# Attention, then a routed expert layer, then a dense layer on one core: two expert tiles filled from six batches run beside the last routing, and expert 0's weights are split inside the attention loop

## The reference, cut to what matters

```
scores = scale * x @ state.T ; a = softmax(scores) ; xread = a @ state
scores2 = scale * state @ x.T ; a2 = softmax(scores2) ; sread = a2 @ x
x = rows of concatenate([xread, sread]) : 4352 x 512

logits = normalise(x) @ normalise(expert_emb).T / tau
expert_idx = argmax(logits) ; gate_w = softmax(logits)[expert_idx]
for e in range(8):
    h = maximum(x[mask_e] @ w1[e], 0)
    out[mask_e] = gate_w * (h @ w2[e])

h = x @ w_in ; r = maximum(h, 0) ; out = (s * r * r + b) @ w_out
```

## Time and profile before

| | |
|---|---|
| median of 3 runs | 1479.9 us (1479.68 to 1480.39) |
| the profiled execution | 1480.5 us |
| its span, first to last instruction | 1478.8 us |
| granted TensorE clock, mean | 0.965 of full speed |
| tiles of the expert stage | 38 |

### The profile page before, as it was taken

How to read it: one execution, slowest core, us unless ns; L and a number is a source line. 1 busy time by engine, 2 the same in 40 slices (tenths; PEclk the granted TensorE clock), 3 DMA queues, 4 the chain that set the end, 5 groups by cost and what they waited for, 6 DMA issues and landing times.

```text
span 1478.8 us, 22719 instructions
## 1 busy us (share of the span) xinstructions
PE 1365.8 (92%) x6878; PEld 1118.7 (76%) x6879; DVE 651.3 (44%) x1646; ACT 509.1 (34%) x977; POOL 149.0 (10%) x196
## 2 busy tenths in 40 slices
PE   5887459999999999997999999999999999999995
PEld 4655338877787877876888888888888888888884
DVE  4776653566664466465632422423223232322322
ACT  3544413455453355353422222222222222222221
POOL 1222310000000000004000100101001010100101
PEclk9988669999999999999999999999999999999998
DMA  9745333144433144214010010101001010010000
GB/s 218 147 112 79 65 106 120 51 150 172 172 115 101 44 161 146 80 52 153 24 44 0 24 34 0 57 0 57 0 0 57 0 57 0 21 36 0 29 1 28
DMA packets 75154, 100.19 MB, mean 68 GB/s; under 512 B 43977, under 2 KB 44521, under 8 KB 74097
## 3 DMA queue, kind: packets, MB, share of 16 engines
q1 hardware_dynamic: 62448, 69.72, 16.7%
q0 software_dynamic: 7200, 20.08, 4.1%
q10 hardware_dynamic: 5472, 9.96, 1.8%
HBM read 71.24 MB, written 28.66 MB: 68 GB/s over the span
## 4 chain that ended last, share of the span: by engine, by line
PE 74%; DVE 7%; DMA 5%; issue 5%; ACT 3%; DVEq 2%; ACTq 1%; POOL 1%; SPq 0%; another core or an unknown queue 0%; POOLq 0%
PE bank_a L1357 25%; PE bank_n L1376 13%; PE bank_t L1376 12%; PE bank_a L1290 9%; PE bank_n L1316 8%; DMA xg<-x_tok,g_idx 3%; PE bank_t L1301 1%; DMA slot_tab<-ids,pos 1%; DMA x_tok<-st_rows 1%; DVEq L339 1%; PE bank_a L1102 1%; PE bank_n L1276 1%; DVEq L336 1%; PE bank_t L1119 1%; DVE w_lo L970 1%
## 5 line engine op out<-in xcount | busy, mean ns | idle before, releaser
L1054 DVE TENSOR_TENSOR sq<-rel 128x512 f32<-128x512 f32 (+1 forms) x144 | 95.5, 663 | 484.8 <-ACT rel L714 484.8
L714 ACT ACTIVATE rel<-bank_a 128x512 f32<-128x512 f32 (+1 forms) x144 | 82.8, 575 | 549.6 <-PE bank_a L1357 549.6
L1357 PE MATMUL bank_a<-y_hi,w_in_hi 128*128 128x512 f32 (+1 forms) x576 | 218.6, 379 | 7.1 <-DVE y_lo L1046 7.0
L1357 PE MATMUL bank_a<-y_hi,w_in_lo 128*128 128x512 f32 (+1 forms) x576 | 217.9, 378 | 0.0
L1357 PE MATMUL bank_a<-y_lo,w_in_hi 128*128 128x512 f32 (+1 forms) x576 | 217.8, 378 | 0.0
L1357 PEld LDWEIGHTS bank_a<-y_hi,w_in_hi 128*128 128x128 f32 x576 | 109.0, 189 | 28.7 <-DVE y_lo L1046 7.5
L1357 PEld LDWEIGHTS bank_a<-y_lo,w_in_hi 128*128 128x128 f32 x576 | 109.0, 189 | 20.7 <-issue 0.2
L1357 PEld LDWEIGHTS bank_a<-y_hi,w_in_lo 128*128 128x128 f32 x576 | 108.9, 189 | 19.9
L1316 PE MATMUL bank_n<-w_hi,hid_hi 128*128 128x512 f32 x304 | 118.4, 389 | 1.9 <-DVE hid_lo L977 1.9
L1316 PE MATMUL bank_n<-w_hi,hid_lo 128*128 128x512 f32 x304 | 118.3, 389 | 0.0
L1376 PE MATMUL bank_n<-wo_hi,g_hi 128*128 128x512 f32 x288 | 112.6, 391 | 0.2 <-DVE g_lo L1057 0.2
(11 more groups left out here) (202 smaller groups left out, 2065.7 us busy)
## 6 DMA issues: line engine op xcount, KB each, us to landing
w_raw<-in_moe_w SPq DMA_DIRECT2D x16, 2048.0 KB, 9.3
moe_tok<-yg ACTq DMA_DIRECT2D x38, 256.0 KB, 2.0
x_tok<-x_rows SPq DMA_DIRECT2D x8, 1088.0 KB
x_m<-in_x SPq DMA_DIRECT2D x8, 1024.0 KB
y_rows<-moe_tok SPq DMA_DIRECT2D x8, 1024.0 KB
win_raw<-in_moe_w_in SPq DMA_DIRECT2D x8, 512.0 KB, 8.9
w_raw<-in_moe_w_out SPq DMA_DIRECT2D x1, 4096.0 KB
slot_tab<-ids,pos POOLq DMA_INDIRECT x40
```

The source lines that it names most:

```text
L714: nc.scalar.activation(rel[:, k, 0:cols], ps_g[k][:, 0:cols], ACT.Relu).then_inc(rel_ready, 1)
L1054: nc.vector.tensor_tensor(sq[:, 0:cols], rel[:, k, 0:cols], rel[:, k, 0:cols], ALU.mult).then_inc(sq_ready, 1)
L1357: last = nc.tensor.matmul(ps_g[n % 2][:, 0:cols], w[:, wc], a[:, c, 0:cols], start=(c == 0 and w is w_in_hi and a is y_hi), stop=(c == DC ...
```

## The change

The changed kernel does four things.

1. **Two early tiles.** Tiles 0 and 1 are filled with the first 256 slots of expert 0 as they stand after batches 0 to 5. SP reads these 256 words (`idx_soon`) after it has stored batch 6, POOL gathers tiles 0 and 1 before it writes the slots of batch 7, and PE, ACT and DVE do these tiles between the steps of the last routing. A correction (`room`, `late`, `first_e`) keeps the table right where expert 0 has fewer than 256 tokens so far; with these inputs `room` is 0 and there are 38 tiles as before. `place` has three more small steps at batch 6 and one more at batches 6 and 7.
2. **Expert 0's weights.** `split_hi(i)` and `split_lo(i)` stand in iteration i of the attention loop, one quarter of w1 or w2 in each, on ACT behind the exponential of `e1` and on DVE behind the quotient of `e1`.
3. **The order of a tile.** DVE does `gate_scale(g+2)` straight after `x_lo(g+2)`, where it did `gate_scale(g+3)` behind `hidden_lo(g+1)`; `gate_final` comes last. The split of `w_in` moves from `next_w1` to `next_w2` on ACT and DVE, and SP loads w2 ahead of `w_in`. SP loads `w_out` after the first `y_rows` and not before them.
4. **Setting up.** POOL writes the constants `first_e` and `late` with four small memsets, and DVE waits for them (`tab_zero`, 8) ahead of the loop.

The diff, cut to its core:

```diff
@@ gpsimd @@
             pool.wait_ge(tab_zero, 4)
             pool.wait_ge(tab_cleared, 16)
-            for bb in range(B):
+            nc.gpsimd.memset(first_e[:], 0.0).then_inc(tab_zero, 1)
+            pool.wait_ge(tab_zero, 5)
+            nc.gpsimd.memset(first_e[:, 0:1], 1.0).then_inc(tab_zero, 1)
+            nc.gpsimd.memset(late[:], 1.0).then_inc(tab_zero, 1)
+            pool.wait_ge(tab_zero, 7)
+            nc.gpsimd.memset(late[:, 0:EARLY], 0.0).then_inc(tab_zero, 1)
+
+            def write_slots(bb):
                 pool.wait_ge(pos_ready, bb + 1)
...
+            for bb in range(B - 1):
+                write_slots(bb)
+            pool.wait_ge(soon_loaded, 16)
+            pool.wait_ge(rows_stored, 16 * SOON)
+            pool.wait_ge(st_stored, 16 * SOON)
+            gather(0)
+            gather(1)
+            write_slots(B - 1)
             pool.wait_ge(rows_stored, 16 * B)
             pool.wait_ge(st_stored, 16 * B)
+            pool.wait_ge(tab_ready, 1)
             pool.wait_ge(idx_ready, 1)
...
@@ vector @@
             dve.wait_ge(const_ready, CONSTS + 2)
             dve.wait_ge(hot_zero, 4)
+            dve.wait_ge(tab_zero, 8)
             for i in range(B):
...
                 nc.vector.tensor_tensor(e1_r, e1_r, r1[:].unsqueeze(2).to_broadcast([P, TPB * H, NS]), ALU.mult)\
                     .then_inc(a1_norm, 1)
+                split_lo(i)
                 if i >= 1:
                     state_logits(i - 1)
                     choose(i - 1)
...
             place(B - 2)
             token_rows(B - 1)
             state_logits(B - 1)
+            dve.sem_inc(hid_t_ready, HB)
+            gate_logits(0)
+            x_lo(0)
             choose(B - 1)
+            gate_scale(0)
             place(B - 1)
+            gate_logits(1)
+            x_lo(1)
+            hidden_lo(0)
+            gate_final(0)
...
+            gate_scale(1)
+            hidden_lo(1)
+            next_w1(1)
+            gate_logits(2)
+            x_lo(2)
+            gate_final(1)
+            gate_scale(2)
+            gate_logits(3)
+            gate_final(2)
+            x_lo(3)
...
             def tile(g):
                 x_lo(g + 2)
+                gate_scale(g + 2)
                 next_w1(g + 1)
-                gate_final(g + 2)
                 gate_logits(g + 3)
                 hidden_lo(g + 1)
-                gate_scale(g + 3)
                 next_w2(g)
-
-            tile(0)
-            with dve.Fori(1, last) as g:
+                gate_final(g + 2)
+
+            with dve.Fori(2, last) as g:
                 tile(g)
@@ scalar @@
                 nc.scalar.activation(e1[:], e1[:], ACT.Exp, scale=-1.0).then_inc(e1_done, 1)
+                split_hi(i)
                 if i >= 1:
                     row_t_evac(i - 1)
...
-            for k in range(2 * WS):
-                split_hi(k)
...
+            x_hi(0)
             gate_square(0)
-            x_hi(0)
             gate_soft(0)
-            act.wait_ge(tab_ready, 1)
             gate_square(1)
             hidden(0)
             x_hi(1)
-            next_w1(0)
+            hidden_hi(0)
+            hidden(1)
+            act.wait_ge(st_stored, 16 * B)
+            result(0)
+            act.wait_ge(tab_ready, 1)
+            store(0)
+            hidden_hi(1)
+            next_w1(1)
+            x_hi(2)
             gate_soft(1)
             gate_square(2)
-            hidden_hi(0)
+            result(1)
+            store(1)
+            gate_soft(2)
+            gate_square(3)
+            hidden(2)
...
@@ tensor @@
             turn_x(0)
-            up(0)
+            up(0, last_ranks)
+            turn_hidden(0)
             turn_x(1)
+            up(1)
+            down(0, turn_slots)
+            turn_hidden(1)
+            down(1, lambda: turn_x(2))
             pe.wait_ge(tab_ready, 1)
+            up(2)
+            turn_x(3)
             last_g = last_tile(pe)
-            tile(0)
-            with pe.Fori(1, last_g) as g:
+            with pe.Fori(2, last_g) as g:
                 tile(g)
@@ sync @@
+                if bb == SOON:
+                    sp.wait_ge(slots_written, 16 * (TPB + 1) * SOON)
+                    with nc.allow_non_contiguous_dma(reason="one word per row"):
+                        sp.dma_start(idx_soon[:], slot_tab[0:EARLY * P, :].rearrange("(t p) o -> p (t o)", p=P)).then_inc(soon_loaded, 16)
...
             sp.wait_ge(tab_ready, 1)
-            sp.wait_ge(gathered, 16)
+            sp.wait_ge(gathered, 16 * (EARLY + 1))
+            sp.wait_ge(st_stored, 16 * B)
             load_win(0)
             for e in range(1, E):
                 sp.wait_ge(w1_ready, WS * e)
                 sp.dma_start(w_raw[:, 0:WCOLS], w1[e].rearrange("(c p) n -> p c n", p=P)).then_inc(w1_loaded, 16)
+                sp.wait_ge(w2_ready, WS * e)
+                sp.dma_start(w_raw[:, WCOLS:2 * WCOLS], w2[e].rearrange("(c p) n -> p c n", p=P)).then_inc(w2_loaded, 16)
                 sp.wait_ge(win_ready, e)
                 load_win(e)
-                sp.wait_ge(w2_ready, WS * e)
-                sp.dma_start(w_raw[:, WCOLS:2 * WCOLS], w2[e].rearrange("(c p) n -> p c n", p=P)).then_inc(w2_loaded, 16)
```

More of the change, by code:

```diff
@@ L503, in _ @@
             gather(3)
-            with pool.Fori(1, last) as g:
+            gather(4)
+            with pool.Fori(2, last) as g:
                 gather(g + 3)
@@ L655, in result @@
                     act.wait_ge(moe_stored, 16 * g)
[L656 removed]
+                nc.scalar.activation(yg[:], ps_y0 if starts(g) else ps_y, ACT.Copy, scale=gate_s[:, ds(g, 1)]).then_inc(yg_ready, 1)
             def store(g):
@@ L685, in tile @@
                 next_w2(g)
-            tile(0)
-            with act.Fori(1, last) as g:
+            with act.Fori(2, last) as g:
                 tile(g)
@@ L1021, in _ @@
+            gate_final(3)
             last = last_tile(dve)
@@ L1302, in turn_hidden, with down @@
                     last.then_inc(hid_tr, 1)
-            def down(g):
-                e = 0 if starts(g) else expert_of(pe, g)
-                if not starts(g):
+            def down(g, between=None):
+                e = 0 if isinstance(g, int) and g < EARLY else expert_of(pe, g)
+                if starts(g):
+                    pe.wait_ge(pos_ready, B)
+                elif not (isinstance(g, int) and g < EARLY):
                     pe.wait_ge(yg_ready, g)
+                dst = ps_y0 if starts(g) else ps_y
                 for w, done, factors in ((w2_hi, w2_hi_done, (hid_hi, hid_lo)), (w2_lo, w2_ready, (hid_hi,))):
+                    if between and w is w2_lo:
+                        between()
                     for k in range(FC):
```

226 lines of the change are left out of this document (129 added, 97 removed).

## The result

| | before | changed |
|---|---|---|
| median, us | 1479.8 (1479.1 to 1480.4, 4 runs) | 1494.9 (1493.0 to 1496.1, 4 runs) |
| ratio | | 1.0101, 95% interval 1.0083 to 1.0118 |
| span of the profiled execution, us | 1478.8 | 1494.4 |

The changed kernel is slower by 15.1 us. The forecast was 7.6 us slower, 1488, with a range up to 1495: the sign was right and the size half of what came. The time lies 0.1 us inside that range by luck, outside the 1483 to 1492 of the likeliest case, and near the 1494 at which the last rival was to be looked for.

A forecast was written before the change was run, and what follows sets the result against it. PE nearly full in the expert tiles, partly idle in the last routing; an engine-to-engine chain sets the attention loop's end. 13.1 + 4.9 - 11.4 + 1 + 0 = +7.6 us gave 1488, range 1478 to 1495.

The forecast's parts named there:

- likeliest case: Whole kernel: the forecast sum of +7.6 us holds, 1488 us, own range 1483 to 1492; chance 0.58.
- last rival: Whole kernel: everything late goes badly, +21 us or 1501, looked for half way at 1494; chance 0.16 (above 1492).
- Part 1: Loop start: first `nb` waits for `tab_zero`, behind the zeros in `slot_tab`; +13.1 us, ends 12 and 14.5.
- Nothing of that moves: Start: SP issues the zeros at 25.50 and they land at 33.2 as before, its stream unchanged up to there.
- Part 2: Attention loop: expert 0's weight quarters cost ACT time on the path, DVE's are free; +4.9 us, ends 2.9 and 6.8.
- Part 3: Last routing: with the early tiles `up(3)` begins at 230.0, not 241.4; -11.4 us, ends 17.7 and 8.0 won.
- Part 4: Expert tiles: new order costs 0.15 us more at each change of expert, +1 us in all; ends -17 and +5.
- The rival that the stalls vanish: Changes of expert: stalls at `w_lo` on DVE go, 17 us less, 1469.5 us; chance 0.11.
- Part 5: End: `gate_scale` beside POOL's adds delays the last `down`, what follows is shorter by the same; 0 us, ends -4 and +3.
- the seven paid quarters: Attention loop, in the rival where everything goes badly: all seven ACT quarters are on the path, 6.8 us.

The follow-up runs named there:

- version with the early gather: Changed kernel with early memsets, old `gate_scale` place, splits in the last routing's waits, `idx_soon` read before batch 6's store, gather 0 before batch 6's slots: ratio 0.9927.

## Why the prediction was right or wrong

| part | predicted, us | trace | alone on the chip, us |
|---|---|---|---|
| 1, the start | +13.1 | `nb` 11.0 later | +14.8 (12.1 to 17.5) |
| 2, the splits in the loop | +4.9 | with part 1: 19.4 at the loop's end | +2.4 (-0.1 to 5.0) |
| 3, the last routing | -11.4 | -11.1 to `up(3)`, -9.7 to `turn_hidden(3)` | -8.3, or -4.9 (worked out) |
| 4 and 5, tiles and end | +1 | +4.6 in the tiles, +1.3 behind them | +5.3 (3.4 to 7.4) |
| sum | +7.6 | +15.6 | 14.2, or 17.6; the whole measured 15.1 and 16.8 |

**Part 1** was right in its mechanism: the zeros in `slot_tab` release the loop. The 13.1 us lie in the measured interval, and the delay counted from `s_t` is 12.7. "Nothing of that moves" was wrong: in all eight traces of kernels built on the changed one the zeros are issued at 23.0 to 24.1 us and the first `s_t` is copied at 18.8 to 19.8, in the six of kernels built on the one before at 25.3 to 25.7 and 20.2 to 21.2. That is a gain of 1.6 us on average that no part had; its cause is open.

**Part 2** has the right place, ACT's path into `x_rows`. Its size was 2.5 us too high on the chip, inside an interval that reaches up to 5.0. A single trace can't check it: the loop from the first `nb` to the last store took from 141 to 157 us in the traces without a late start, with or without splits. That parts 1 and 2 together gave 18.0 and the trace 19.4 is for the same reason no proof of either.

**Part 3.** In the first trace the steps end where they were put: in the clock of before, shifted by 19.4 us, the first gather lands at 175.7 (175.5 predicted), `up(3)` begins at 230.3 (230.0). The first of these was luck. The gather was priced at an issue at 169.2 and 6.3 us; it was issued at 166.75, 2.4 earlier, and took 9.0. The three other traces with this routing show 9.2 to 10.6 us from the issue to `turn_x(0)`. From the last store to `turn_hidden(3)` the four took 72.8, 75.0, 75.1 and 78.2 us, six with the old routing 80.7 to 83.7: the first pair of traces shows more than most, and 8.3 or 4.9 on the chip is less than 11.4, with the 1.6 us of the earlier start still in them. What was missed besides is that `up(3)` still runs at the lower clock and needs 6.9 us, and loses 1.4 of the gain before `turn_hidden(3)`. The one buffer `xg` showed as a wait before both `turn_x(3)` and `turn_x(4)`, 1.45 and 2.76 us and not 4 to 7 in one. By the Trainium skill (DMA: Bandwidth & Descriptors, Queues, rings and completion order) the increment of the gather's semaphore can't land before the earlier writes of its DMA engine. The last slots were issued at 184.81; with the 8.64 us of before their landing would be at 193.45, an estimate, and the gather landed at 195.17. That agrees with the rule and doesn't test it, since the rows themselves moved until 194.8.

**Part 4 is the step that failed.** It said that a change of expert would cost 0.15 us more, 1 us in all; the traces show 4.6. PE's wait for `w_lo` went, as said, but no single new wait for `xg_lo` took its place: the gather and `hid_lo` are each a little late in three tiles, and of the 4.6 us `w_in`'s new place makes 3.1, `gate_scale`'s 1.5. The working counted DVE and ACT up to `x_lo` and left out that `gate_logits` stands behind `next_w1`, and that a later `lg` is a later gather. The rival that the stalls vanish was wrong: in both new places that were tried, `gate_scale` delays something else by more than `w_lo` gains.

**Part 5** named the mechanism and both ends and took the middle. On the way to the first dense product 2.5 us are lost, near the upper end of 3; of these 1.1 come back in the dense stage. By the Trainium skill (GPSIMD Engine Reference, Specifications; the prediction names a section that the page doesn't have) GpSimd contends with VectorE instructions of two SBUF inputs, so the slowness goes with `gate_scale` to its new place. The trace agrees: 10.1 us beside the adds in the new place, 9.2 in the old one, 3.3 without them. To give that rule the value zero in the sum was a choice against the evidence.

Between the predicted sum and that of the measured parts lie 6.6 us (14.2 - 7.6): parts 4 and 5 make 4.3, part 3 makes 3.1 (6.5 by the other value), and parts 1 and 2 nearly cancel (1.7 - 2.5). The last rival, everything late goes badly, had a chance of 0.16 and comes nearest. Its start of 14.5 (14.8), its 8.0 of the routing (8.3) and its 5 in the tiles (4.6 in the trace) came; the seven paid quarters, 6.8, did not (2.4).

The version with the early gather is faster than both kernels: 10.8 us less than before, 0.9927. It keeps the early tiles, has nothing new at the start and splits no weights in the loop. It was not tried with `w_in`'s split back in its old place, which by the tiles would win 3 us more.

## What to carry to other kernels

A constant that is written behind a wait on the engine that writes it makes every reader wait for that too; four memsets of 0.1 us cost 15 us here. Work moved into a wait of one engine must be looked at from the engine beside it: POOL's adds and DVE's operations on two SBUF operands slowed each other in both places where they were laid side by side, and DVE's `w_lo` lengthened POOL's DMA issues while keeping its own 4.63 us. A stall that is taken from a loop with three coupled engines is gained only if what is moved delays nothing else on any of them; here it was spread over the next tiles. A step that comes out on time in one trace should be checked in its parts: the first gather was early by 2.4 us and slow by 2.7.

## What the hardware showed

- POOL's issue of an indirect DMA took 0.97 us by itself and 1.7 to 2.0 beside `w_lo` (two fp32 operands of 128x1024 in SBUF).
- Beside POOL's adds of 128x512 on SBUF, DVE's `wo_lo` took 1.44 us in place of 0.62, `sq` 1.48 in place of 0.42, and a `gate_scale` of 3.3 us took 9.2 and 10.1. Its one-column steps with a constant kept their 0.15 us. POOL's own add took 1.37 us on average beside `gate_scale` and 1.53 beside `wo_lo`, where the one that ran before them took 1.29.
- After PE had stood for some 12.7 us at the start, the first stretch ran at a granted clock of 0.69, 0.80 and 0.81 in three traces; in those without the stand it was 0.84 to 0.93.
- A gather of 128 rows moved its 0.28 MB in 1.1 to 1.6 us when no large store ran beside all of it, and in 7 us behind five slot DMAs with the store of 1088 KB beginning beside it.
